# Attention with weighted sums of 65 streamed columns in place of 130

## The reference, cut to what matters

```python
scores = scale * np.matmul(q, k.transpose(0, 1, 3, 2))
kth = np.partition(scores, -top_k, axis=-1)[..., -top_k:-top_k + 1]
scores = np.where(scores >= kth, scores, -1000000000.0)
scores = scores - np.max(scores, axis=-1, keepdims=True)
attn = np.exp(scores)
attn = attn / (np.sum(attn, axis=-1, keepdims=True) + 1e-09)
return np.matmul(attn, v).astype(np.float32)
```

## Time and profile before

| what | value |
|---|---|
| median of 3 runs | 1054.71 us (1053.94 to 1055.05) |
| profiled execution, span from first to last instruction | 1053.0 us; its time is not listed apart from the span, which lies 1.7 us below the median |
| TensorE busy, share of the span | 950.2 us, 90% |
| VectorE busy | 781.8 us, 74% |
| ScalarE busy | 621.8 us, 59% |
| GpSimd busy | 616.4 us, 59% |
| mean granted TensorE clock | 0.980 of full |

### The profile page before, as it was taken

The page is one execution under the profiler, slowest core; times in us unless marked ns, Lnnn a source line. Parts: engine busy times, 40 slices in busy tenths (PEclk is TensorE's granted clock), DMA queues, the critical chain, the costliest instruction groups (busy, mean ns, idle before and its releaser), DMA issues.

```text
span 1053.0 us, 20897 instructions
## 1 busy us (share of the span) xinstructions
PE 950.2 (90%) x6238; PEld 669.4 (64%) x6238; DVE 781.8 (74%) x1515; ACT 621.8 (59%) x1269; POOL 616.4 (59%) x932
## 2 busy tenths in 40 slices
PE   3899999999998999999999989996799999999995
PEld 1566666666666666666666666342487788777884
DVE  5999999999999999999999993107625543554251
ACT  2788888788888888878888873102413432433121
POOL 3577777777777777777777770102435454554452
PEclk9999999999999999999999998998799999999998
DMA  9911210210110110110110016999724434433332
GB/s 345 421 63 35 70 37 12 70 47 5 67 48 14 57 48 14 58 48 14 57 48 14 2 42 223 374 421 423 323 33 116 118 51 113 114 41 42 43 40 32
DMA packets 24947, 109.03 MB, mean 104 GB/s; under 512 B 3328, under 2 KB 4768, under 8 KB 17696
## 3 DMA queue, kind: packets, MB, share of 16 engines
q1 hardware_dynamic: 17040, 87.82, 21.9%
q0 software_dynamic: 7104, 11.18, 8.2%
q10 hardware_dynamic: 720, 8.98, 2.3%
HBM read 88.35 MB, written 16.07 MB: 99 GB/s over the span
## 4 chain that ended last, share of the span: by engine, by line
PE 34%; DVE 29%; issue 19%; POOL 7%; DMA 5%; ACT 3%; DVEq 1%; SPq 0%; POOLq 0%; ACTq 0%
PE psum L971 14%; DVE arena L1244 8%; PE psum L976 7%; DVE arena L1240 5%; DVE arena L1232 5%; DVE arena L1228 4%; POOL arena L1555 3%; DVE arena L1236 3%; DMA arena<-w_top 3%; DVE arena L1248 2%; ACT h_hi L1204 2%; PE psum L584 2%; POOL arena L1588 2%; DMA arena<-xs_rows,arena 2%; PE psum L958 1%
## 5 line engine op out<-in xcount | busy, mean ns | idle before, releaser
L1555 POOL TENSOR_SCALAR arena<-arena 128x576 bf16<-128x576 f32 x144 | 249.6, 1733 | 134.9 <-DVE arena L1228 128.4
L627 PE MATMUL psum<-arena 128*128 128x130 f32 x1550 | 215.1, 280 | 0.0
L627 PEld LDWEIGHTS psum<-arena 128*128 128x128 f32 x1550 | 180.3, 179 | 33.9 <-issue 4.8
L584 PE MATMUL psum<-arena 64*128 64x288 f32 (+1 forms) x640 | 111.9, 462 | 57.7 <-DVE arena L1236 52.1
L1514 DVE COPY arena<-psum 128x512 f32 x41 | 28.3, 691 | 153.6 <-PE psum L976 135.0
L1204 ACT ACTIVATE h_hi<-psum 128x512 fp32r<-128x512 f32 x80 | 43.4, 595 | 161.2 <-PE psum L958 161.2
L971 PE MATMUL psum<-w_hi,h_hi 128*128 128x512 f32 x320 | 131.9, 412 | 6.8 <-ACT h_hi L1204 2.0
L999 ACT ACTIVATE arena<-arena 128x576 bf16<-128x576 bf16 x144 | 98.6, 685 | 51.3 <-POOL arena L1555 50.9
L971 PE MATMUL psum<-w_lo,h_hi 128*128 128x512 f32 x320 | 127.4, 398 | 0.0
L1678 POOL DMA_INDIRECT out<-arena x40 | 64.2, 1605 | 95.5 <-ACT arena L1186 67.2
L1232 DVE MAX8 arena<-psum 128x8 f32<-128x576 f32 x144 | 109.2, 758 | 11.7 <-PE psum L596 11.2
(11 more groups left out here) (240 smaller groups left out, 1634.8 us busy)
## 6 DMA issues: line engine op xcount, KB each, us to landing
weights<-w_soft SPq DMA_DIRECT2D x21, 1024.0 KB, 17.1
arena<-qkv SPq DMA_DIRECT2D x15, 864.0 KB, 4.5
weights<-w_top SPq DMA_DIRECT2D x12, 1024.0 KB, 25.9
arena<-w_soft SPq DMA_DIRECT2D x11, 1024.0 KB, 8.5
weights<-w_top SPq DMA_DIRECT2D x3, 2048.0 KB, 27.7
weights<-w_top ACTq DMA_DIRECT2D x3, 2048.0 KB, 7.9
arena<-qkv SPq DMA_DIRECT2D x16, 325.0 KB, 3.0
out<-arena SPq DMA_DIRECT2D x1, 4864.0 KB, 18.7
```

The source lines that it names most:

```text
L584: last = nc.tensor.matmul(bank(2 * (t % 2) + x, SH)[q0:q0 + rows, :], qT[u][half, w * P + q0:w * P + q0 + rows], kT[u][half, h * SH:(h + 1 ...
L627: last = nc.tensor.matmul(o_place(n, k)[0:rows, :], wT[0:kr, t % 2, kc, q0:q0 + rows], v_, start=(kc == 0), stop=(kc == KC - 1))
L1555: nc.gpsimd.tensor_scalar(hit[t % 2], s_sb[t % S_SLOTS], m8[t % S_SLOTS][:, 7:8], None, ALU.is_ge) \
```

## The change

An output of 128 rows streams the 65 columns of its own head, as the others do, and the outputs of a duo lie 65 columns apart in bank 7.

```diff
         def o_widths(n):
-            return [2 * VW if rows == P else VW for _, rows, *_ in duo_outputs(n)]
+            return [VW for _ in duo_outputs(n)]
...
         def o_wanted(n, k0, k1, rows):
 
-            starts = [sum(o_widths(n)[0:k]) + (VW * h if rows == P else 0)
-                      for k, _, _, h, *_ in duo_outputs(n)[k0:k1]]
+            starts = [sum(o_widths(n)[0:k]) for k in range(k0, k1)]
...
                     for kc in range(KC):
                         kr = P if kc < NC else REM
-                        v_ = vv[u][0:kr, kc, :, :].rearrange("p h w -> p (h w)") if rows == P else vv[u][0:kr, kc, h, :]
-                        last = nc.tensor.matmul(o_place(n, k)[0:rows, :], wT[0:kr, t % 2, kc, q0:q0 + rows], v_,
-                                                start=(kc == 0), stop=(kc == KC - 1))
+                        last = nc.tensor.matmul(o_place(n, k)[0:rows, :], wT[0:kr, t % 2, kc, q0:q0 + rows],
+                                                vv[u][0:kr, kc, h, :], start=(kc == 0), stop=(kc == KC - 1))
```

## The result

The changed kernel takes 1082.61 us, median of four runs (1075.25 to 1084.69), against 1054.8 before (also four runs): a ratio of 1.0264 with a 95% interval of 1.0241 to 1.0287, 27.8 us slower. It was forecast to be slower by 63 us, at 1118. The profiled run is the quickest of the four, 1075.25 us with a span of 1073.4; it is 20.4 us longer than the span of before. The attention stage holds all of that: VectorE reads the strike of the last iteration's tile 14 (L1230, L1232 before) at 631.4 us in place of 610.9.

The account below looks back on a forecast made before the run. VectorE was taken to set the pace in the attention stage. To the 1053.0 us span came +64 for clock falls and 0 for freed PE time, 1117; with the median 1.7 above the span, 1118 us, range 1065 to 1265.

Parts of the forecast that it names:

- What bounds it: Attention stage, 36 to 635 us: VectorE sets the pace, TensorE has about 0.6 us of slack per round.
- Price of a pass: Weighted sums (L627): loads set the spacing, so only 0.18 us a pair of outputs is saved, 11 us of PE time.
- The 68 us: Weighted sums: estimated saving if moving columns alone spaced the matmuls, halving 1250 passes; the prediction sided against it.
- Freed time worth zero: Attention stage: the 11 us of PE time saved shorten the path by zero, bounds 0 and -4.6 us.
- The clock falls: Attention stage: narrow bursts joined by idle time repeatedly lower TensorE's clock, +64 us, bounds +10 and +210; chance 0.82.
- the fall at 639 us: Kernel before, after L711's 65-column work: clock 0.50 from 639.30 to 649.30 us without a PE pause, read as the sign.
- 29 x 2.2 = +64 us: Attention stage: 29 low stretches in 70 rounds, each taken as 6 us long and costing 2.2 us.
- The price per low microsecond: Attention stage: a low stretch of 6 us was taken to cost 2.2 us, bounds 1.0 and 3.
- the work that had restored the clock at 35 us: Kernel before: scores, a strike and transposes run without a pause, after which the clock level rose; every round has them.
- The clock did not hold: Rival for the attention stage: surrounding work keeps the clock full, 1054.7 us less at most a few tenths; chance 0.09.
- No freed time reached VectorE: Rival for the attention stage: 3.1 of VectorE's 4.6 us late waits go at full clock, 1051.6 us; chance 0.05.
- The clock did not stay low: Rival: the clock falls and stays low for the attention stage, +315 to +490, so 1370 to 1545 us; chance 0.04.

Follow-up runs that it names:

- 97 columns: Kernel before with full outputs streaming 97 of the pair's 130 columns: 1054.12 us, ratio 0.9997.
- the two kernels that split the duos: 65 columns only in duos 0, 3, 4, 5 and 8, or only in 1, 2, 6 and 7, 130 in the others: 1061.49 and 1075.45 us.
- run 14: Not a run's label: the words read "In the profiled run", then "14 of the 16 stretches"; that is the changed kernel's profiled run, 1075.25 us.
- both edits: Kernel before with six 512-column fillers around the first strikes and 130 columns in full outputs of the last two duos: 1052.45 us.

## Why the prediction was right in kind and wrong in size

**What bounds it** held: VectorE sets the pace, and 97 columns show that PE time alone is worth nothing.

**Price of a pass** held: twenty loads 2.73 us in the changed kernel, as read at L711. (The 68 us given beside it halve the measured pass; 65 columns at 2.4 GHz are 0.027 us a record, so the estimate should be 34 us. The sum uses neither.) **Freed time worth zero** held.

**The clock falls** held, and the reading it rested on, the fall at 639 us with PE busy throughout, stands as far as the attention stage goes: the same form brought 16 falls there, and four fillers inside the burst or 97 columns took all or all but one away. In the place of that reading itself it is less firm: 130 columns left no fall, but 65 did so too in three traces. The Trainium skill (Perfetto Trace Analysis, Identifying the Most-Contended Engine) trusts the share of weight loads more than that of matmuls as a measure of how near PE is to its limit. Neither gave a sign of the clock here: both shares of the span are the same before and after (64% and 90%), and ahead of the fall at 639 us the loads were busy 3.03 of 3.30 us.

**The step that failed** is the sum "29 x 2.2 = +64 us": the number of low stretches and the 6 us taken for each. The profiled run has 16 of 3.8 us on average, 61 us low against 29 x 6 = 174. The price per low microsecond was nearly right: 20.4 us lost over 61 us is 0.33, against 2.2 / 6 = 0.37 forecast. (By the time at which the last tile 14 is read it is 0.35 to 0.37 in the two kernels that split the duos, and 0.47 in the narrow one with six fillers.) By the mean clock the slower runs of the changed kernel fit the same price: at 0.94 in place of 0.95 some 21 us more are low, five or six stretches, which at 0.33 is 7 us, and the median lies 7.4 us above the profiled run. So about 22 stretches stand against 29, and 3.8 us against 6: the length was missed by more than the number.

The length I took between two rows, though the work that had restored the clock at 35 us follows every burst at once; the clock mostly rose after 3.4 us. The number was a guess of two in five over all 70 bursts. In the profiled run 14 of the 16 stretches follow the 31 bursts of duos 1, 2, 6 and 7, and two the other 39; over all runs the split by duos gives those four about twice the low time of the rest. What in these steps does it is open.

**The rivals.** The clock did not hold, though four fillers inside the burst make it hold. No freed time reached VectorE. The clock did not stay low; the nearest to it is the narrow kernel with six fillers, with 30 falls.

## What to carry to other kernels

A matmul whose time is set by its weight loads streams extra columns nearly free of charge (0.18 us a duo here), and here those columns kept TensorE's clock. So look at the granted clock behind bursts of narrow matmuls before you trim them; the busy share ahead of the falls, 3.06 and 3.30 of 3.30 us, warned of nothing. In this kernel filler work was best put inside the burst as wider streams (1054.8 us), not as instructions of its own (1059.85), which stand in the queue ahead of work that others wait for. Where a trace already runs the new form somewhere, even in one corner, read both its price and what the clock did behind it, and in more than one run: the fall at 639 us was there in some traces and not in others.

## What the runs showed that was not expected

Filler matmuls can make things worse: three more per step, 8 us under wide sums, were 29 us under narrow ones (1082.61 to 1111.37), with 30 falls for 16. The spread of the runs grew as well: from 1.1 us in four runs before (6.6 us in the widest set of 17) to 9.4 us in four of the changed kernel and 13.4 us in six with 65 columns in duos 0, 3, 4, 5 and 8, so how many falls a run gets differs from run to run. And raising the clock earlier gave back what it gained: with 3.3 us less waiting in the first 35 us, PE paused 1.88 us at each of two turns of the loop, and the clock fell there. Versions without fillers and with both edits show the same two places. The clock then falls under 130 columns as well, so these columns guard against the falls behind the bursts and not against an idle PE; and a change in PE's list of instructions can bring such a pause, which shows only in its order of time.
